# Expert weights handled in pairs of chunks: one 512 KB transfer, one rounding and one subtraction of 128x1024 for two chunks

## The reference, cut to what matters

```python
logits = xc @ w_gate
e_idx = np.argmax(logits, axis=1)
...
for e in range(E):
    mask = e_idx == e
    h = np.maximum(xc[mask] @ w1[e], 0.0)
    y[mask] = gate_w[mask, None] * (h @ w2[e])
out[do_compute] = xc + y
```

## Time and profile before

| | before |
|---|---|
| median of 3 runs, us | 712.0 (707.68 to 713.35) |
| the profiled execution, us | 714.29 |
| its span, first to last instruction, us | 712.7 |
| TensorE matmul busy | 662.6 us, 93% |
| VectorE busy | 392.0 us, 55% |
| ScalarE busy | 356.6 us, 50% |
| GpSimd busy | 170.1 us, 24% |
| subtractions of chunks, line 1005 | 96 and 64 of 128x512, means 717 and 683 ns |
| roundings of chunks, line 820 | 96 and 64 of 128x512, 57.4 us for the first 96 |
| HBM traffic | 116 GB/s over the span |

### The profile page before, as it was taken

The page is one execution under the profiler, slowest core; times in us unless marked ns, Lnnn a source line. Parts: engine busy times, 40 slices in busy tenths (PEclk is TensorE's granted clock), DMA queues, the critical chain, the costliest instruction groups (busy, mean ns, idle before and its releaser), DMA issues. The chain is left out here.

```text
span 712.7 us, 13052 instructions
## 1 busy us (share of the span) xinstructions
PE 662.6 (93%) x4457; PEld 566.4 (79%) x4458; DVE 392.0 (55%) x1374; ACT 356.6 (50%) x1025; POOL 170.1 (24%) x204
## 2 busy tenths in 40 slices
PE   3889999999999999999999999999978989897993
PEld 3568888888888889899889898988856767686772
DVE  4767774556456434343343342435655887687862
ACT  4778766656656433333333333334442764656650
POOL 5335421232223102000010010100305453055431
PEclk9999999999999999999999999999988999999997
DMA  7448635323321240102002001012335764676630
GB/s 255 155 132 261 215 103 169 104 78 128 108 73 40 77 165 22 69 1 89 1 1 88 0 30 59 0 60 69 94 119 167 238 226 143 216 248 215 216 129 13
DMA packets 45154, 81.53 MB, mean 114 GB/s; under 512 B 6594, under 2 KB 10690, under 8 KB 45088
## 3 DMA queue, kind: packets, MB, share of 16 engines
q1 hardware_dynamic: 41360, 75.01, 32.1%
q0 software_dynamic: 3184, 4.64, 2.2%
q10 hardware_dynamic: 544, 1.05, 0.4%
HBM read 65.06 MB, written 17.47 MB: 116 GB/s over the span
## 5 line engine op out<-in xcount | busy, mean ns | idle before, releaser
L1427 PE MATMUL ph<-x_hi,w_hi 128*128 128x256 f32 x576 | 165.9, 288 | 1.2 <-DVE x_lo L1066 1.2
L1161 DVE SCALAR_TENSOR_TENSOR gated<-gated,ph 128x256 f32<-128x256 f32 x144 | 60.6, 421 | 188.2 <-ACT gated L897 188.1
L1427 PE MATMUL ph<-x_lo,w_hi 128*128 128x256 f32 x576 | 160.5, 279 | 0.0
L1427 PE MATMUL ph<-x_hi,w_lo 128*128 128x256 f32 x576 | 160.4, 278 | 0.0
L1440 PE MATMUL px<-w_hi,g_hi 128*128 128x512 f32 x288 | 118.0, 410 | 0.0
L1427 PEld LDWEIGHTS ph<-x_hi,w_hi 128*128 128x128 f32 x576 | 108.2, 188 | 8.3 <-issue 3.3
L1440 PE MATMUL px<-w_hi,g_lo 128*128 128x512 f32 x288 | 114.0, 396 | 0.0
L1440 PE MATMUL px<-w_lo,g_hi 128*128 128x512 f32 x288 | 113.3, 394 | 0.0
L1427 PEld LDWEIGHTS ph<-x_lo,w_hi 128*128 128x128 f32 x576 | 108.7, 189 | 3.6
L1427 PEld LDWEIGHTS ph<-x_hi,w_lo 128*128 128x128 f32 x576 | 108.7, 189 | 0.0
L897 ACT ACTIVATE gated<-ph 128x256 f32<-128x256 f32 x144 | 54.9, 381 | 102.3 <-PE ph L1427 102.3
(11 more groups left out here) (216 smaller groups left out, 1062.9 us busy)
## 6 DMA issues: line engine op xcount, KB each, us to landing
w_raw<-we SPq DMA_DIRECT2D x64, 256.0 KB, 3.5
more_raw<-we SPq DMA_DIRECT2D x64, 256.0 KB, 4.3
w_raw<-wf SPq DMA_DIRECT2D x32, 256.0 KB, 3.7
vs<-vw SPq DMA_DIRECT2D x16, 384.0 KB, 3.2
qs<-qT SPq DMA_DIRECT2D x16, 288.0 KB, 4.0
ks<-kT SPq DMA_DIRECT2D x16, 288.0 KB, 4.6
xT_dram<-x_stage SPq DMA_DIRECT2D x16, 288.0 KB, 3.1
x_lo<-xT_dram SPq DMA_DIRECT2D x8, 512.0 KB, 3.5
```

What stands on the lines that cost most here:

```text
L1161: nc.vector.scalar_tensor_tensor(gated[s % 2][:, :], gated[s % 2][:, :], 1.0, ph[s % 2][:, 0:TT], ALU.add, ALU.mult).then_inc(gated_done, 1)
L1427: last = nc.tensor.matmul(ph[f % 2][:, 0:TT], up_w(w, k, f), x[p][:, k, :], start=(at == 0 and n == 0), stop=(at == KD - 1 and n == 2))
```

## The change

Experts 1 to 7 (and the conditional tiles) go by pairs of chunks. SyncE waits for both chunks of the pair four pairs back and issues one transfer of 512 KB; ScalarE rounds 128x1024 in one instruction, VectorE subtracts 128x1024 in one. Semaphores count two for a pair. The places in the hand-written order are dealt anew. Expert 0 and the dense layer are as before.

```diff
+        def two_chunks(w, p, c):
+            at = p * ECH + (2 * c if p else 2 * c % KD * (FB // GF) + 2 * c // KD)
+            return w[:, :].rearrange("p (n s) -> p n s", s=CH)[:, at:at + (2 if p else FB // GF + 1):(1 if p else FB // GF), :]
...
-        FIRST_NEXT = 6
+        FIRST_NEXT = 3
...
+            def load_pairs(e, t):
+                for c in range(ECH // 2):
+                    sp.wait_ge(w_lo_done, NCH + t * ECH + 2 * c + 2 - ERAW)
+                    sp.dma_start(two_raw(c), we[bass.ds(e, 1), 2 * c:2 * c + 2, :, :].rearrange("a c p s -> p (a c) s")).then_inc(w_raw_in[2 * c % ERAW], 16)
+
             for t in range(1, E):
-                load_expert(t, t, range(ECH))
+                load_pairs(t, t)
...
+            def pair_hi(t, p, c):
+                at = 2 * c % ERAW
+                act.wait_ge(w_raw_in[at], 16 * ((NCH // RAW if at < RAW else 0) + t * (ECH // ERAW) + 2 * c // ERAW + 1))
+                nc.scalar.activation(two_chunks(w_hi, p, c), two_raw(c), ACT.Copy).then_inc(w_hi_done, 2)
...
                 relu(t, 0, 0)
-                next_hi(0, 1, 2)
+                next_hi(0)
                 relu(t, 0, 1)
                 split_h_hi(t, 0, 0)
                 relu(t, 1, 0)
                 split_h_hi(t, 0, 1)
-                next_hi(3, 4, 5)
+                next_hi(1, 2)
                 relu(t, 1, 1)
                 split_h_hi(t, 1, 0)
-                next_hi(6, 7, 8)
+                next_hi(3)
                 split_h_hi(t, 1, 1)
-                next_hi(9, 10)
+                next_hi(4)
                 if more:
                     xe_split_hi(t + 1, 1 - p)
-                next_hi(11, 12, 13, 14, 15)
+                next_hi(5, 6, 7)
...
+            def pair_lo(t, p, c):
+                dve.wait_ge(w_hi_done, NCH + t * ECH + 2 * c + 2)
+                nc.vector.tensor_tensor(two_chunks(w_lo, p, c), two_raw(c), two_chunks(w_hi, p, c).bitcast(F32),
+                                        ALU.subtract).then_inc(w_lo_done, 2)
...
                 split_h_lo(t, 0, 0)
-                next_lo(0, 1, 2)
+                next_lo(0)
                 split_h_lo(t, 0, 1)
-                next_lo(3, 4, 5)
+                next_lo(1, 2)
                 sum_h(t, 0)
-                next_lo(6)
+                next_lo(3)
                 split_h_lo(t, 1, 0)
-                next_lo(7)
                 sum_h(t, 1)
-                next_lo(8)
+                next_lo(4)
                 split_h_lo(t, 1, 1)
                 if more:
                     xe_split_lo(t + 1, 1 - p)
                 both_rows()
                 if isinstance(t, int) and t == META_TILE:
                     find_more_tiles()
-                next_lo(9, 10, 11, 12, 13, 14, 15)
+                next_lo(5, 6, 7)
```

More of the change, by code:

```diff
@@ L419, in e_down_w, with two_raw @@
             return w[:, e_chunk(p, EUPCH + f)]
+        def two_chunks(w, p, c):
+            at = p * ECH + (2 * c if p else 2 * c % KD * (FB // GF) + 2 * c // KD)
+            return w[:, :].rearrange("p (n s) -> p n s", s=CH)[:, at:at + (2 if p else FB // GF + 1):(1 if p else FB // GF), :]
+        def two_raw(c):
+            slot = 2 * c % ERAW
+            return w_raw[:, slot:slot + 2, :] if slot < RAW else more_raw[:, slot - RAW:slot - RAW + 2, :]
         def raw(slot):
@@ L583, in _ @@
             load_expert(0, 0, range(ERAW, ECH))
+            def load_pairs(e, t):
+                for c in range(ECH // 2):
+                    sp.wait_ge(w_lo_done, NCH + t * ECH + 2 * c + 2 - ERAW)
+                    sp.dma_start(two_raw(c), we[bass.ds(e, 1), 2 * c:2 * c + 2, :, :].rearrange("a c p s -> p (a c) s")).then_inc(w_raw_in[2 * c % ERAW], 16)
             for t in range(1, E):
-                load_expert(t, t, range(ECH))
+                load_pairs(t, t)
             def load_more(o):
                 e = sp.value_load(meta[0:1, bass.ds(o, 1)], min_val=0, max_val=E - 1)
-                load_expert(e, o + E, range(ECH))
+                load_pairs(e, o + E)
             sp.wait_ge(meta_done, 1)
@@ L959, in _, with next_hi @@
             split_h_hi(0, 0, 1)
-            for ch in range(FIRST_NEXT):
-                expert_hi(1, 1, ch)
+            for c in range(FIRST_NEXT):
+                pair_hi(1, 1, c)
             xe_split_hi(0, 0, [1])
             def routed_tile(s, p, t, more=True):
-                def next_hi(*chunks):
-                    for ch in chunks if more else ():
-                        expert_hi(t + 1, 1 - p, ch)
+                def next_hi(*pairs):
+                    for c in pairs if more else ():
+                        pair_hi(t + 1, 1 - p, c)
                 if is_first(t):
                     relu(t, 1, 0)
-                    next_hi(*range(FIRST_NEXT, 9))
+                    next_hi(*range(FIRST_NEXT, 5))
                     relu(t, 1, 1)
@@ L975, in routed_tile @@
                     xe_split_hi(t + 1, 1 - p)
-                    next_hi(*range(9, ECH))
+                    next_hi(*range(5, ECH // 2))
                     return
                 relu(t, 0, 0)
-                next_hi(0, 1, 2)
+                next_hi(0)
                 relu(t, 0, 1)
@@ L1264, in _ @@
             nc.vector.memset(py[1][:, :], 0.0).then_inc(py_cleared, 1)
-            for ch in range(FIRST_NEXT):
-                expert_lo(1, 1, ch)
+            for c in range(FIRST_NEXT):
+                pair_lo(1, 1, c)
             xe_split_lo(0, 0, [1])
@@ L1308, in routed_tile, with next_lo @@
             def routed_tile(s, p, t, more=True):
-                def next_lo(*chunks):
-                    for ch in chunks if more else ():
-                        expert_lo(t + 1, 1 - p, ch)
+                def next_lo(*pairs):
+                    for c in pairs if more else ():
+                        pair_lo(t + 1, 1 - p, c)
                 def add_rows(h, at=0, to=None):
@@ L1330, in routed_tile @@
                 if is_first(t):
-                    next_lo(*range(FIRST_NEXT, 9))
+                    next_lo(*range(FIRST_NEXT, 5))
                     for o in range(EFO):
@@ L1335, in routed_tile @@
                     xe_split_lo(t + 1, 1 - p)
-                    next_lo(*range(9, 12))
+                    next_lo(5)
                     both_rows()
-                    next_lo(*range(12, ECH))
+                    next_lo(6, 7)
                     return
                 split_h_lo(t, 0, 0)
-                next_lo(0, 1, 2)
+                next_lo(0)
                 split_h_lo(t, 0, 1)
-                next_lo(3, 4, 5)
+                next_lo(1, 2)
                 sum_h(t, 0)
-                next_lo(6)
+                next_lo(3)
                 split_h_lo(t, 1, 0)
-                next_lo(7)
                 sum_h(t, 1)
-                next_lo(8)
+                next_lo(4)
                 split_h_lo(t, 1, 1)
```

## The result

| | before | after |
|---|---|---|
| median, us | 708.4 (8 runs, 706.8 to 713.4) | 717.9 (8 runs, 713.2 to 718.5) |
| ratio of the times | | 1.0111, 95% interval 1.0086 to 1.0135 |
| the profiled execution, us | 714.29 | 717.76 |
| its span, us | 712.7 | 716.2 |
| VectorE busy, us | 392.0 | 389.5 |

The change makes the kernel 1.1% slower, though both helpers do less: the forecast of 711.7 (707 to 716) was wrong. More runs lowered the median of before as well: in 35 runs it is 708.8, and the execution profiled before was one of its slower ones.

A forecast was written before the change was run, and what follows sets the result against it. TensorE is busy nearly throughout; in the routed layer its waits, chiefly tile 3's 6 us, were the target. Terms 0.8 + 1.1 + 0.9 - 2.4 - 0.7 = -0.3 us gave 711.7 us, range 707 to 716.

The forecast's parts named there:

- What a pair costs: 128x1024 instructions: a pair lasts 1.25 us on VectorE, 1.05 on ScalarE, and takes 1.16 and 0.94 of their time.
- Tile 0: First sum waits for whole pairs: +0.8 us; TensorE's idle of 0.44 becomes 1.4, with no clock fall costed.
- Tile 1: From `h_lo` to TensorE on the split tokens 12.7 us instead of 11.6, pair 4's rounding standing behind `h_rest`: +1.1 us.
- Tiles 2, 4, 6: Same alternating work with TensorE busy beside it; last `h_rest` makes TensorE 0.3 us late, three times: +0.9 us.
- the ladder: VectorE and ScalarE alternating from `h_lo` through sums, `h_rest` and pairs to the split tokens; 12.7 us in tile 1.
- Tile 3: Pair 4 subtracted early removes 6.3 us of waiting; later waits leave 23.5 us for 27.2, clock fall 1.3: net -2.4.
- Tile 5: VectorE's run after the rows is three pairs instead of seven chunks, so GpSimd's addition ends 0.7 us earlier: -0.7.
- the third: Rival: slower, pair 4 behind `h_rest`, pairs as dear as two chunks, clock falls in tile 0; +3.0, 715 us, chance 0.25.
- The fourth: Rival: the stall only moves; a pair lands after 5.5 us, tile 3's fourth `relu` 1.9 later; 713.6 us, chance 0.10.
- the second: Rival: the cure wins; pairs at 1.08 and 0.85 us, no clock fall after tile 3; -4.0, 708 us, chance 0.25.

The follow-up runs named there:

- e3: Changed kernel's order, but every pair is two single chunks again, in transfers and instructions; 708.2 us, ratio 0.9989 to before.
- e9: Changed kernel's order and 128x1024 instructions, but transfers of 256 KB instead of 512 KB; 717.0 us, ratio 1.0111 to before.
- e1: Changed kernel with pair 4 rounded on ScalarE ahead of the second split of half 1; 707.0 us, ratio 0.9972 to before.
- e0: The kernel before, unchanged, run and profiled again; 709.0 us, ratio 0.9998 to before.
- e5: Kernel before with chunks 9 and 10 subtracted ahead of the rows and of `find_more_tiles`; 703.0 us, ratio 0.9915 to before.
- e13: e3 with chunks 8 and 9 rounded ahead of the last `h_rest`; 703.4 us, ratio 0.9923 to before.
- e6a: Changed kernel without the branch ahead of tile 7 and the conditional part for more tiles; 713.7 us, ratio 1.0047 to before.
- e12: Changed kernel with pair 4 rounded ahead of the last `h_rest` and subtracted behind the split of the tokens; 706.5 us, ratio 0.9954 to before.
- e2: Changed kernel with pair 4 subtracted on VectorE only behind the split of the tokens; 706.9 us, ratio 0.9971 to before.

## Why the prediction was wrong, step by step

Lengths of the tiles, each from the start of its first matmul to that of the next tile:

| tile | before, two profiles | after | e3 | forecast | measured, against the two |
|---|---|---|---|---|---|
| 1 | 18.4, 18.4 | 19.6 | 18.9 | +1.1 | +1.2 |
| 2 | 22.9, 22.9 | 24.5 | 22.7 | +0.3 | +1.6 |
| 3 | 27.2, 26.5 | 24.9 | 23.2 | -2.4 | -2.3, -1.5 |
| 4 | 21.2, 21.2 | 21.8 | 21.2 | +0.3 | +0.6 |
| 5 | 20.1, 19.5 | 20.0 | 18.9 | -0.7 | -0.1, +0.5 |
| 6 | 22.4, 22.5 | 25.0 | 23.3 | +0.3 | +2.6, +2.5 |

Against the first profile, from which the forecast was made, tiles 1 to 6 were to be 1.1 us shorter in all and are 3.7 longer. Of these 4.8 us tile 6 has 2.3 and tile 2 has 1.3. Nearly every sign that the forecast named came: the durations of pairs, a tile 3 of 23 to 25 us, 3.5 us or more ahead of tile 2, the short idles of tiles 2, 4 and 6. What they lead to was priced wrong.

- **What a pair costs: right.** 1.22 and 1.05 us measured, 1.25 and 1.05 forecast. For VectorE the estimate by the Trainium skill (VectorE: DVE Perf Modes, section on the TRN2 errata), 1.22, is the closer one for the duration; of two back to back, which take 2.34, the second adds 1.12, near the 1.16 of the rows, and on ScalarE 0.95, near 0.94.
- **Tile 0: right in what was late, wrong in the clock.** The idle ahead of `py` is 1.15 us (1.4 forecast). The text took no fall of the clock behind it, "shorter than the shortest behind which the clock fell"; it had fallen there (0.53, below). The old kernel has its fall in the same tile a few us earlier, so in this profile it costs nothing net. From the first matmul of the second half's tokens to the start of tile 1 it is 13.0 us, 11.9 before: +1.1 for the +0.8 of the forecast, with another 0.79 us of idle, ahead of `phT`, that it didn't have.
- **Tile 1: right**, as said above.
- **Tiles 2, 4, 6: the step that failed.** It took the ladder against TensorE's need of `h_rest` and found 0.3 us late. The idle there is indeed 0.34, 0.33 and 0.34. What was left out is what a late `h_rest` is passed on to. In tile 6 it is the branch ahead of tile 7, where the idle went from 0.93 to 2.91 us, and +0.3 became +2.6, the largest single miss; without the branch tile 6 takes 21.9 us in the changed kernel and 21.3 in the old one. The forecast quoted the 0.93 us ahead of tile 7 as "for nothing that shows" and then gave tile 6 the price of tile 2, instead of asking why the queue stood still. In tile 2 it is the clock: the 24 matmuls behind the wait took 8.35 us, 7.33 before, as the granted clock stayed at its lower level for 6.8 us and not for 3.4. That is 1.0 of the 1.6. It fell during the 4.63 us of idle ahead of tile 2, not behind tile 2's own `h_rest`, and of the four profiles with these instructions and 4.3 to 4.7 us of idle there one, e9, has it low for 3.4 us: there tile 2 takes 23.3, +0.4 for the forecast's +0.3.
- **Tile 3: mechanism right, 1.4 us too hopeful in its length.** 24.9 us, 23.5 forecast. ScalarE waits at pairs 1 and 2 as forecast, but pair 2's transfer landed 4.7 us after its slot was free, not 3.6, so `relu` came 1.04 us late (0.3 forecast), and the late sums brought 0.35 and 1.49 (1.8 forecast). The 3.6 came from rows of transfers into `w_raw`, and pair 2 goes into `more_raw`, for which the page of before gives a median of 4.3 already at 256 KB. The fall of the clock costed at 1.3 didn't come, and the two errors cancel: that the tile's -2.4 was met is luck.
- **Tile 5: half right.** GpSimd's addition shrank from 4.17 us to 3.36 as forecast. What it won was lost where TensorE ran the next twelve matmuls: 5.35 us, as the clock stayed low for 6.8 us; before they took 4.15, with 3.4 us low.

The chain of the changed kernel's tile 3 (start, us, what) and GpSimd in tile 5:

```profile
606.39 1.22 DVE w_lo L1221
607.62 4.72 DMA more_raw<-we
612.47 0.92 issue
613.39 0.59 ACT relu_h L949
```

```profile
647.77 3.36 POOL L684 TENSOR_TENSOR tick<-tick 1x1 f32<-1x1 f32 x1 [0.73 <-DVE rows L1340]
```

The granted clock of the changed kernel (third number from the end) in tile 0's `py`, at the start of tile 2 and four us on, in tile 5, and in tile 3:

```profile
549.50:551.50 2.00, 1.56 (x4) 1.31 (x5) 1.46 (x4) 1.07 (x4) 1.16 (x2) 0.53 0.59 215
575.00:577.00 2.00, 2.00 (x6) 1.54 (x6) 1.96 (x4) 0.89 (x1) 1.19 (x2) 0.50 0.65 239
578.00:580.00 2.00, 2.00 (x7) 1.54 (x6) 2.00 (x3) 0.00 (x0) 2.00 (x1) 0.50 0.39 105
662.00:664.00 2.00, 2.00 (x6) 1.55 (x5) 0.79 (x1) 2.00 (x5) 0.00 (x0) 0.50 0.78 278
608.00:612.00 4.00, 3.86 (x20) 2.95 (x19) 3.97 (x5) 1.36 (x2) 0.00 (x0) 1.00 0.94 307
```

From 540 us to TensorE's last matmul the changed kernel has three low stretches, of 3.4, 6.8 and 6.8 us, 17 us in all at 1.2 GHz; both profiles of before have four of 3.4, 13.6 us, and e1 and e3 have two of 3.4, 6.8 us. Other than four was one of the forecast's own signs of being wrong.

**Of the rivals** the third named the right place, pair 4 behind `h_rest`, with a chance of 0.25 and 715 us. Its reason was wrong: it made pairs dear, and they are not. With pairs at their forecast price the ladder already costs this much, since the loss is the grain, which e3 against e9 shows: same order, same work, 8.9 us between the medians. The fourth was in part right, by the 4.7 us of pair 2's transfer, and the second's cheap pairs (1.08) weren't seen.

**What stays open.** The medians of before and after lie 9.5 us apart, the spans of e0 and of the changed kernel 7.2. About 2 us of the difference is that e0's profiled execution (its span and 1.6 us, so 710.6) is itself slower than the median. Of the 7.2, 4.8 are in the tiles and 2.3 ahead of tile 1, where the change touches only tile 0: tile 1 starts at 552.8 us in e0 and at 555.1 and 555.3 in the two profiles of the changed kernel, but at 549.9 in e9, whose clock has no fall in tile 0. One or two profiles for each kernel can't tell such scatter from an effect; the two of before lie 2.5 us apart at this place. So only about half of the 9.5 us, the 4.8 in the tiles, is traced to a place. Nor was it tried whether e5's move and e13's add up.

## What to carry to other kernels

Where two engines hand work to each other, merging two instructions saved a little time on each here and added half an instruction of waiting at every handover; count the handovers on the path first, and merge only where neither engine waits for the other. Look ahead of each merged instruction for work on the path that now stands behind it: here one such instruction, moved by one place, was worth 10 us. And a short idle that the profile can't explain can be a long latency with its cover half gone, as ahead of the branch here: find what feeds the queue ahead of it before pricing a delay there. If a change brings two things, price its useful half alone; here (e5) that was one move of two chunks.

## What the runs showed of the hardware

- A register read and a branch over the code of the conditional part cost 4.5 to 5.4 us from the last wait ahead of them to the first matmul behind, hidden only as far as queued matmuls reach, and in all 12 profiles a 16 KB transfer of instructions lies in this time. A read and a branch inside a tile took at most 2.3 to 2.6 us from wait to matmul, all of it hidden.
- Between 500 us and the last matmul every low stretch of the granted clock lasted 3.4 or 6.8 us. The wait ahead of it doesn't tell whether one comes or how long it is: behind 1.15 us in tile 0 one came in the changed kernel and in e6a, and none in e9 and e12; behind 4.63 us ahead of tile 2 it lasted 6.8 us, behind 4.70 in e9 3.4, behind 3.68 in e2 6.8; in tile 5 it lasted 6.8 us behind a wait of 2.06 for the gather and 3.4 behind 3.10 in the old kernel; behind 2.91 ahead of tile 7 none came, behind 2.45 in e9 one did.
- A tiny addition of GpSimd beside a run of VectorE's subtractions lasts about as long as the run: 4.17 us beside seven chunks, 3.36 beside three pairs. Beside the five chunks of e5 it took 2.36 and ended one chunk before them, so it isn't always the last.
